# Later zeros, earlier rows: reordered loads and scatters in a fused attention, MoE and MLP kernel

## The reference

```
scores = q k^T / 8 + bias(head, distance), causal window of 128   (2 batches, 8 heads, 576, 64)
x      = softmax(scores) v                      -> 1152 x 512
e(i)   = argmax(x w_gate); gate = softmax(x w_gate)[e(i)]
         each of 8 experts keeps its first 288 tokens, the others give 0
y(i)   = gate * relu(x w1[e]) w2[e]             w1: 8 x 512 x 1024, w2: 8 x 1024 x 512
out    = (h * sigmoid(h)) w_out, h = y w_in     w_in: 512 x 2048
```

## Time and profile before

| what | us |
|---|---|
| median of 3 runs | 451.75 |
| the profiled execution | 454.15 |
| its span | 452.0 |
| PE busy | 435.0 (96%) |
| DVE, ACT, POOL busy | 213.6, 220.1, 230.0 |

### The profile page before, as it was taken

One profiled execution on the slowest core, in us unless ns is written; L12 is line 12 of the kernel. 1 busy time (PEld: TensorE's weight loads), 2 busy tenths in 40 slices (PEclk: granted clock), 3 DMA queues, 4 the chain that ended last, 5 costly groups with the idle time before them and its releaser, 6 DMA issues.

```text
span 452.0 us, 8317 instructions
## 1 busy us (share of the span) xinstructions
PE 435.0 (96%) x2928; PEld 396.2 (88%) x2928; DVE 213.6 (47%) x728; ACT 220.1 (49%) x547; POOL 230.0 (51%) x172
## 2 busy tenths in 40 slices
PE   7999899998999999999999999999999999999995
PEld 5787677788999999999999999988999989999983
DVE  4687687786375574765763222131222231312230
ACT  5878588655576666666675543221312222212221
POOL 5005778578978989889799987402000002000002
PEclk9999999998999999999999999999999999999999
DMA  9998992139977768887878200001000001000002
GB/s 170 255 285 219 263 279 62 50 112 331 339 263 280 265 222 250 291 306 244 292 265 269 105 1 1 2 0 70 1 0 0 0 0 70 0 0 0 0 0 75
DMA packets 54247, 63.70 MB, mean 141 GB/s; under 512 B 32064, under 2 KB 32064, under 8 KB 54208
## 3 DMA queue, kind: packets, MB, share of 16 engines
q1 hardware_dynamic: 51392, 58.23, 42.1%
q0 software_dynamic: 1776, 4.73, 2.9%
q10 hardware_dynamic: 1040, 0.26, 0.3%
HBM read 53.76 MB, written 9.44 MB: 140 GB/s over the span
## 4 chain that ended last, share of the span: by engine, by line
PE 73%; SPq 9%; POOL 6%; DMA 4%; ACT 3%; DVE 2%; issue 2%; POOLq 0%
PE bank L1324 15%; PE bank L1325 14%; PE bank L1326 14%; PE bank L1346 13%; SPq L344 7%; PE bank L1345 6%; POOL w_lo L502 5%; PE bank L1343 2%; DMA q_raw<-in_q_dram 2%; DMA dispatched<-dispatch_dram 2%; PE bank L1154 2%; PE bank L1193 1%; PE bank L1171 1%; PE bank L1205 1%; PE bank L1344 1%
## 5 line engine op out<-in xcount | busy, mean ns | idle before, releaser
L502 POOL TENSOR_TENSOR w_lo<-w_raw,w_hi 128x1024 fp32r<-128x1024 f32 x72 | 171.2, 2412 | 22.2 <-DVE w_lo L1074 9.4
L1105 DVE TENSOR_TENSOR bank<-bank,sigmoid 128x384 f32<-128x384 f32 x48 | 27.2, 567 | 135.8 <-ACT sigmoid L755 135.8
L755 ACT ACTIVATE sigmoid<-bank 128x384 f32<-128x384 f32 x48 | 23.6, 492 | 127.3 <-PE bank L1326 127.3
L602 POOL DMA_INDIRECT out_dram<-out_stage,permcol x9 | 8.8, 974 | 150.9 <-ACT out_stage L775 149.8
L661 ACT ACTIVATE w_hi<-w_raw 128x1024 fp32r<-128x1024 f32 x76 | 80.1, 1054 | 2.4 <-DMA w_raw<-in_moe_w_dram 2.4
L1034 DVE TENSOR_REDUCE bank<-bank 128x192 f32<-128x384 f32 (+5 forms) x96 | 49.2, 514 | 44.6 <-PE bank L1346 44.3
L1324 PE MATMUL bank<-x_hi,w_hi 128*128 x192 | 65.0, 338 | 0.7 <-POOL w_lo L502 0.7
L1326 PE MATMUL bank<-x_hi,w_lo 128*128 x192 | 64.6, 336 | 0.0
L1325 PE MATMUL bank<-x_lo,w_hi 128*128 x192 | 64.5, 336 | 0.0
L1346 PE MATMUL bank<-hidden,w_hi 128*128 128x384 f32 (+5 forms) x224 | 63.0, 354 | 0.0
L1324 PE MATMUL bank<-w_hi,g_hi 128*128 128x512 f32 x144 | 56.7, 394 | 0.8 <-DVE g_lo L1109 0.8
(11 more groups left out here) (154 smaller groups left out, 766.9 us busy)
## 6 DMA issues: line engine op xcount, KB each, us to landing
w_raw<-in_moe_w_dram SPq DMA_DIRECT2D x64, 512.0 KB, 6.2
dispatch_dram<-zeros SPq DMA_DIRECT2D x4, 1152.0 KB, 8.3
w_raw<-in_moe_w_in_dram SPq DMA_DIRECT2D x8, 512.0 KB, 4.7
w_raw<-in_moe_w_out_dram SPq DMA_DIRECT2D x8, 512.0 KB, 6.8
dispatched<-dispatch_dram SPq DMA_DIRECT2D x8, 384.0 KB, 7.7
q_raw<-in_q_dram SPq DMA_DIRECT2D x8, 256.0 KB, 6.9
v_raw<-in_v_dram SPq DMA_DIRECT2D x8, 256.0 KB, 6.5
k_raw<-in_k_dram SPq DMA_DIRECT2D x7, 256.0 KB, 7.9
```

The costliest lines, as they stand in the source:

```text
L502: nc.gpsimd.tensor_tensor(wlo[s][:, sl], raw[s][:, sl], whi[s][:, sl], ALU.subtract).then_inc(pool_lo, 1)
L755: nc.scalar.activation(sig[:, f % 2, :], bank[f % 4][:, 0:TB], ACT.Sigmoid).then_inc(sig_ready, 1)
L1105: nc.vector.tensor_tensor(bank[f % 4][:, 0:TB], bank[f % 4][:, 0:TB], sig[:, f % 2, :], ALU.mult).then_inc(gf_ready, 1)
```

## The change

- The fourth zero write is issued behind q, k and v of block 5 instead of ahead of them.
- POOL scatters block 7 ahead of `select_first` of block 8, block 8 right behind that, and block 9 alone behind the wait for the last slots. Before, all three came behind both.
- The plan is made in three parts. DVE makes ranks, counts and expert numbers, then `excess`, then row 1 of `plan` (expert numbers). Row 0 (offsets), with `kept_above`, moves behind the lows of the first rows, into `output_places`; ACT and DVE wait for it as `plan_ready` 3. `above` moves from SBUF to a bank of PSUM.
- SP, which needs row 1 only, loads one piece of the second expert's w1, waits for the scatters, loads that expert's rows, then the third block of slots, then the other pieces.
- POOL makes 7 pieces of every expert but the first, DVE one. The wait for DVE's piece of the expert before stands ahead of piece 0, for the last expert ahead of piece 1.
- In the MLP `g_high(f)` and `g_low(f)` follow `sigmoid(f)` and `g_full(f)` directly; in the first block the high piece stands between `sigmoid(f)` and `g_high(f)`.
- In the narrow version PE no longer waits for the third block of slots in the first expert.

```diff
@@ SP, block.sync
-            empty_slots(2 * NT - 4, E - 2 * NT + 4)
             for t in range(NT, NTOK):
                 sp.wait_ge(pv_done, 2 * (t - NT + 2))
                 load_qkv(t)
+                if t == NT:
+                    empty_slots(2 * NT - 4, E - 2 * NT + 4)
...
             sp.wait_ge(xd_in, 16)
-            load_w1(expert[1], 2, range(2))
+            load_w1(expert[1], 2, range(1))
             sp.wait_ge(scattered, 16 * NTOK)
-            load_third(0)
             sp.wait_ge(step_done, KC)
             load_dispatched(expert[1])
-            load_w1(expert[1], 2, range(2, PIECES))
+            load_third(0)
+            load_w1(expert[1], 2, range(1, PIECES))
             load_w2(expert[1], 3)
@@ POOL
+            pool.wait_ge(xd_in, 16)
+            scatter(LAST)
             pool.wait_ge(seen_ready, NTOK)
             select_first(LAST + 1)
-            pool.wait_ge(xd_in, 16)
+            scatter(LAST + 1)
             pool.wait_ge(last_slots, NTOK - LAST)
-            for t in range(LAST, NTOK):
-                scatter(t)
+            scatter(LAST + 2)
...
             def lows(e, w_slot, pieces):
                 for p in pieces:
+                    if e >= 2 and p == (1 if e == E - 1 else 0):
+                        pool.wait_ge(dve_lo, e - 1)
                     low_here(w_slot + p // PIECES, p % PIECES, split_by(e, p + 1))
@@ ACT, mlp_block
                     sigmoid(tb, f)
-                    if f >= 1:
-                        g_high(tb, f - 1)
                     if first and f < 2 * PIECES:
                         weight_high(2 + f // PIECES, f % PIECES, 16 * (E // 2 + 1))
-                g_high(tb, F2C - 1)
+                    g_high(tb, f)
@@ DVE
-            link(nc.vector.tensor_tensor(ranked[:, 0], at_rank[:], kept8.unsqueeze(1).broadcast_to(over_e), ALU.mult))
-            link(nc.vector.reduce_sum(by_rank[:, 0, :], ranked[:, 0], axis=AX.X))
+            link(nc.vector.tensor_tensor(ranked[:, 0:2], at_rank[:].unsqueeze(1).broadcast_to([P, 2, E, E]),
+                                         vals[:, 0:2].unsqueeze(2).broadcast_to([P, 2, E, E]), ALU.mult))
+            link(nc.vector.reduce_sum(by_rank[:, 0:2], ranked[:, 0:2], axis=AX.X))
...
             nc.vector.tensor_scalar_max(excess[:], over[:], 0.0).then_inc(plan_ready, 1)
-            link(nc.vector.tensor_tensor(kept_above[:], above[:], kept8.unsqueeze(1).broadcast_to(over_e), ALU.mult))
-            link(nc.vector.reduce_sum(off8, kept_above[:], axis=AX.X))
-            link(nc.vector.tensor_tensor(ranked[:, 1:3], at_rank[:].unsqueeze(1).broadcast_to([P, 2, E, E]),
-                                         vals[:, 1:3].unsqueeze(2).broadcast_to([P, 2, E, E]), ALU.mult))
-            link(nc.vector.reduce_sum(by_rank[:, 1:3], ranked[:, 1:3], axis=AX.X))
-            nc.vector.tensor_copy(plan[:], by_rank[:, 1:3, :]).then_inc(plan_ready, 1)
+            nc.vector.tensor_copy(plan[:, 1, :], by_rank[:, 1, :]).then_inc(plan_ready, 1)
             def output_places():
+                link(nc.vector.tensor_tensor(kept_above[:], above, kept8.unsqueeze(1).broadcast_to(over_e), ALU.mult))
+                link(nc.vector.reduce_sum(off_e, kept_above[:], axis=AX.X))
+                link(nc.vector.tensor_tensor(ranked[:, 2], off_e.unsqueeze(1).broadcast_to(over_e), at_rank[:], ALU.mult))
+                link(nc.vector.reduce_sum(off_r, ranked[:, 2], axis=AX.X))
+                nc.vector.tensor_copy(plan[:, 0, :], off_r).then_inc(plan_ready, 1)
                 nc.vector.reduce_sum(droprank, over_c[:], axis=AX.X)
-                link(nc.vector.reduce_sum(off_e, kept_above[:], axis=AX.X))
...
@@ DVE, MLP
                         g_full(tb, f)
-                        if f >= 1:
-                            g_low(tb, f - 1)
-                    g_low(tb, F2C - 1)
+                        g_low(tb, f)
@@ PE, turn and down steps
-                            pe.wait_ge(third_in, 16)
+                            if e > 0:
+                                pe.wait_ge(third_in, 16)
```

More of the change, by code:

```diff
@@ L161, in build @@
     first8, o = at("first_bias", [P, E], F32, o)
-    above, o = at("above", [P, E, E], F32, o)
     kept_above, o = at("kept_above", [P, E, E], F32, o)
@@ L284, in pooled_by @@
         def pooled_by(e, n):
-            return sum(map(pooled, range(e))) + n
-        def pooled(e):
-            return SPLITS if e == 0 else POOLED - 1 if e == E - 2 else POOLED
+            return POOLED * e + n + (1 if e > 0 else 0)
         def low_of(e, kind, c):
@@ L577, in lows @@
                 for p in pieces:
+                    if e >= 2 and p == (1 if e == E - 1 else 0):
+                        pool.wait_ge(dve_lo, e - 1)
                     low_here(w_slot + p // PIECES, p % PIECES, split_by(e, p + 1))
-            lows(1, 2, range(pooled(1)))
+            lows(1, 2, range(POOLED))
             for e in range(2, E):
-                pool.wait_ge(dve_lo, e - 1)
-                lows(e, 2 * (e % 2), range(pooled(e)))
-            pool.wait_ge(dve_lo, E - 1)
+                lows(e, 2 * (e % 2), range(POOLED))
             lows(E, 0, range(2 * PIECES))
@@ L724, in steps @@
                         if e == 0:
-                            act.wait_ge(plan_ready, 2)
+                            act.wait_ge(plan_ready, 3)
                         off = offset_of(act, e)
@@ L992, in _ @@
             dve.wait_ge(count_done, 1)
-            kept8, off8 = vals[:, 0, :], vals[:, 1, :]
+            kept8, expert_no = vals[:, 0, :], vals[:, 1, :]
+            above = bank[COUNTS][:, P:P + E * E].rearrange("p (i j) -> p i j", i=E)
             over_e = [P, E, E]
@@ L1006, in _ @@
             nc.vector.tensor_scalar_max(excess[:], over[:], 0.0).then_inc(plan_ready, 1)
-            link(nc.vector.tensor_tensor(kept_above[:], above[:], kept8.unsqueeze(1).broadcast_to(over_e), ALU.mult))
-            link(nc.vector.reduce_sum(off8, kept_above[:], axis=AX.X))
-            link(nc.vector.tensor_tensor(ranked[:, 1:3], at_rank[:].unsqueeze(1).broadcast_to([P, 2, E, E]),
-                                         vals[:, 1:3].unsqueeze(2).broadcast_to([P, 2, E, E]), ALU.mult))
-            link(nc.vector.reduce_sum(by_rank[:, 1:3], ranked[:, 1:3], axis=AX.X))
-            nc.vector.tensor_copy(plan[:], by_rank[:, 1:3, :]).then_inc(plan_ready, 1)
-            def output_places():
-                off_e, off, droprank, base_ = (bank[COUNTS][:, 16 * n:16 * n + w] for n, w in
-                                               ((1, E), (2, NTOK), (3, NTOK), (4, NTOK)))
+            nc.vector.tensor_copy(plan[:, 1, :], by_rank[:, 1, :]).then_inc(plan_ready, 1)
+            def output_places():
+                off_e, off, droprank, base_, off_r = (bank[COUNTS][:, 16 * n:16 * n + w] for n, w in
+                                                      ((1, E), (2, NTOK), (3, NTOK), (4, NTOK), (5, E)))
+                link(nc.vector.tensor_tensor(kept_above[:], above, kept8.unsqueeze(1).broadcast_to(over_e), ALU.mult))
[3 more added lines that the diff above has]
+                nc.vector.tensor_copy(plan[:, 0, :], off_r).then_inc(plan_ready, 1)
                 nc.vector.reduce_sum(droprank, over_c[:], axis=AX.X)
-                link(nc.vector.reduce_sum(off_e, kept_above[:], axis=AX.X))
                 link(nc.vector.tensor_tensor(oo[:], off_e.unsqueeze(1).broadcast_to([P, NTOK, E]), onehot[:], ALU.mult))
@@ L1062, in steps @@
                         if e == 0:
-                            dve.wait_ge(plan_ready, 2)
+                            dve.wait_ge(plan_ready, 3)
                         off = offset_of(dve, e)
@@ L1071, in steps @@
                     if e >= 1 and (kind, c) == ("up", 1):
[L1072 removed]
+                        s, sl = 2 * (e % 2) + 1, slice((PIECES - 1) * PIECE, PIECES * PIECE)
                         dve.wait_ge(whi_ready, split_by(e, SPLITS))
@@ L1378, in steps @@
                         if c == 0:
-                            pe.wait_ge(pool_lo, pooled_by(e, pooled(e)))
-                            if e > 0:
+                            if e == 0:
+                                pe.wait_ge(pool_lo, SPLITS)
+                            else:
+                                pe.wait_ge(pool_lo, pooled_by(e, POOLED))
                                 pe.wait_ge(dve_lo, e)
```

9 lines of the change are left out of this document (4 added, 5 removed).

## The result

The kernel after takes 448.26 us (median of 20 runs, 447.2 to 453.6) against 452.05 for the kernel before (20 runs, 451.03 to 454.14). The ratio is 0.9927, 95% interval 0.9906 to 0.9948, so 2.4 to 4.3 us faster (3.3 by the ratio itself), where 6.7 was forecast; the medians differ by 3.8. The direction and the range held, the size did not. All medians here are of all runs, while the ratios, and their 95% intervals in brackets, leave out runs that lie over 1.5% above the fastest of their kernel.

The account below looks back on a forecast made before the run. PE was taken as the bound, idle only in a few waits, plus a low-clock stretch; 0.9 + 0.4 + 1.8 + 1.6 - 0.2 + 0.7 + 1.5 = 6.7 us off 451.75 gave 445.05 us, range 443.0 to 448.6.

Parts of the forecast that it names:

- terms 1 and 4: Attention: q of block 6 earlier, 0.9 us; second expert: no low clock behind PE's wait for its rows, 1.6 us.
- Terms 2 and 6: First expert's lows start earlier, 0.4 us; at the MLP's start PE's wait for low pieces goes, 0.7 us.
- Zeros: Attention: with the fourth zero write behind block 5's loads, q of block 6 comes earlier; 0.9 us gained.
- rival A: Attention: by DMA ring order q of block 6 lands when it did, zeros bring nothing; 445.95 us, chance 0.22.
- Scatters and plan: Before the first expert: offsets leave DVE's path, first low and PE start earlier despite later selections; 0.4 us gained.
- The rows' wait: Second expert: rows issued earlier with less traffic behind, PE's wait for them goes; 1.8 us gained.
- The clock: Second expert's transposes and first `down` step: without PE idle ahead, no low clock there; 1.6 us gained.
- terms 2 to 5: From scatters and plan to the second expert: 0.4 + 1.8 + 1.6 - 0.2 = 3.6 us faster.
- Piece 1: Second piece of the second expert's w1, now behind the rows, lands later and ACT stands; 0.2 us lost.
- Rival B: Second expert: w1 pieces land late, ACT, POOL and PE wait, clock falls again; 447.5 us, chance 0.20.
- Start of the MLP: POOL's seven pieces without a wait end PE's wait for low pieces there; 0.7 us gained.
- MLP: At the ends of MLP blocks the gap before PE's last steps goes, 0.5 us three times; 1.5 us gained.

Follow-up runs that it names:

- experiment 4: Kernel before with five added memsets on POOL between the wait for the zeros and the first scatter: 451.54 us, ratio 0.9984.
- experiments 1, 2: Kernel after with the fourth zero write back ahead of block 5: 448.4 us; kernel before with only that write moved behind block 5's loads: 452.65 us.
- experiment 11: Kernel after with POOL's and DVE's w_lo shares and waits as before: 449.49 us; then with the fourth zero write back too: 448.75 us.
- experiment 5: Kernel before, unchanged, profiled a second time: 452.58 us.
- experiment 8: Kernel before with only the new order of scatters, plan and SP's loads: 450.3 us, ratio 0.9945.
- experiment 6: Kernel after, unchanged, profiled a second time: 448.87 us, ratio 0.993 to the kernel before.
- experiment 9: Kernel before with only POOL's seven pieces of every expert but the first, and the new waits for DVE's piece: 452.51 us, ratio 1.0001.

## Why the prediction was wrong in size

The step that failed is the last one of the sum: "This execution is 2.4 above the median, so the runs should come to 451.75 - 6.7". I had noted that the execution was 2.4 us slower than the others and still took its waits off the median. The profile of experiment 4, of a run of 451.57 us, shows what the 2.4 us were. Its span is 2.5 us shorter (449.5): 0.6 in the attention (32.87 instead of 33.44), 0.5 in the wait for the rows (1.31 instead of 1.77), and 1.6 at the low clock (from the transposes to the second expert 119.35 - 109.12 = 10.23 instead of 121.87 - 110.04 = 11.83), less 0.1 elsewhere. So nearly all of terms 1 and 4 was in the 2.4 us already. Terms 2 and 6 were also too large, by 0.2 and 0.5.

1. **Zeros (0.9).** Measured nothing (experiments 1, 2); in experiment 11 the kernel with the zeros back is the faster one by 0.7, within the noise. Even in the profile that it was read from there was less to win: its two waits of 1.32 us made the stretch only 0.60 longer (33.44 against 32.84). The unused 0.26 of the DMA engines is 0.06 in experiment 5: the reason I gave for rejecting rival A was itself a feature of one execution. A's price (term 1 is nothing) came true, though not its reason: q isn't waited for.
2. **Scatters and plan (0.4).** In the first profiles 98.86 - 55.48 = 43.38 became 100.80 - 57.58 = 43.22: 0.2, and 0.2 (43.38 - 43.20) in experiment 8. Selections were late by 0.3 in the first profile (97.51 - 57.58 against 95.09 - 55.48) and by 0.5 in experiment 8, as `select_first` follows a scatter.
3. **The rows' wait (1.8).** Right: gone in all nine profiles with the new order, and 1.3 to 2.3 in the six with the old one, 1.8 on average; that the one profile had just the average is luck.
4. **The clock (1.6).** Right for the profile (66.39 - 62.67 = 3.7 for terms 2 to 5 together, forecast 3.6), wrong for the median: in five other executions nothing was there to be won.
5. **Piece 1 (0.2).** ACT waited 0.28 us for it, 0.83 in experiment 6; PE lost nothing. Rival B did not happen.
6. **Start of the MLP (0.7).** 0.2, for the reason in experiment 9. I took DVE's and POOL's work as independent; at 215.50, where I looked, POOL was waiting for DVE's piece. But another pair of rows of before shows the conflict: DVE's piece at 198.45 takes 1.70 us and ends at 200.15, 1.08 after POOL's (199.07).

```profile
191.96 7.11 POOL L502 TENSOR_TENSOR w_lo<-w_raw,w_hi 128x1024 fp32r<-128x1024 f32 x3
```

```profile
198.45 1.70 DVE L1074 TENSOR_TENSOR w_lo<-w_raw,w_hi 128x1024 fp32r<-128x1024 f32 x1
```
7. **MLP (1.5).** 1.7.

0 + 0.2 + 1.8 + 0 + 0 + 0.2 + 1.7 = 3.9 us, against 3.8 between the medians and 3.3 by the ratio. The terms are from single profiles, so that they meet the 3.8 so closely is in part luck.

## What to carry to other kernels

Profile the kernel before twice, or compare its profiled time with its other runs: when the profiled execution is slow by 2 us, as here, some of its waits can be these 2 us, and then they can't be taken off the median. Before filling an idle stretch of POOL, look at what DVE does in it: with two SBUF inputs on both sides only one of them ran (2.34 us instead of 1.22 for DVE, 3.40 instead of 2.36 for POOL). A result of DVE that PE needs soon should not queue behind back-to-back POOL instructions (DVE's piece, with `hidden` behind it, took up to 7.85 us instead of 1.22, and PE waited 3.7 us).

## What the runs showed that I had not expected

- DVE, kept waiting by POOL, got its turn at the next end of a POOL instruction (2.34 us) or not until POOL had nothing more to do (3.79, 4.68, 4.74, and 7.85 with POOL's instructions half as long). In the one kernel with shorter instructions on POOL it was worse.
- The granted clock behind an idle of PE was 0.50 in some cases (1.52, 1.77, 2.09, 2.68, 2.82 and 5.26 us) and 1.00 in others (1.16, 1.31, 1.35, 1.51, 2.26 and 2.34), and once it fell to 0.50 with no idle above 0.2 us ahead of it.
- One `eqw` of 8 columns took 1.90 us beside POOL's scatter and cast, in one of the six profiles that have the zeros moved and the cast in its place. That is also the profile with the latest first scatter, 20.6 us behind q of block 3, against 17.9 to 18.7 in the other five, so the later zeros may have a part in it. Whether cast or scatter held it stays open.
